# GpSimd starts the work of a head pair after PV of the pair before it, and splits x one pair further back

## The reference

```python
scores = scale * np.matmul(q, k.transpose(0, 1, 3, 2))          # 4 x 8 heads, 576 x 576, head size 64
thresh = np.max(scores, axis=-1, keepdims=True) - tau
scores = np.where(scores >= thresh, scores, -1000000000.0)
attn = np.exp(scores - np.max(scores, axis=-1, keepdims=True))
attn = attn / (np.sum(attn, axis=-1, keepdims=True) + 1e-09)
x = np.matmul(attn, v)                                          # laid out as batch, 576, 512
# token and channel mixing
h = np.maximum(x.transpose(0, 2, 1) @ w_tok1, 0.0) @ w_tok2     # 576 -> 256 -> 576
u = x + h.transpose(0, 2, 1)
y = u + np.maximum(u @ w_ch1, 0.0) @ w_ch2                      # 512 -> 1536 -> 512
# gated convolution
h = np.maximum(y @ w_in, 0.0)                                   # 512 -> 1024
conv_out = ...                                                  # three taps along the sequence
out = h * sigmoid(conv_out) @ w_out
```

## Time and profile before

| what | value |
|---|---|
| median of 3 runs | 849.05 us (848.79 to 851.71) |
| the profiled execution | 850.66 us, of which the span of the trace is 848.9 us |
| PE busy / PEld / DVE / ACT / POOL | 97% / 79% / 50% / 49% / 31% |
| the attention stage | from the start to about 360 us |
| one even and one odd body | 40.1 us, from the first `h1l` at 162.88 us to the first `h1l` at 202.97 us |
| mean granted TensorE clock | 0.997 of full speed |

### The profile page before, as it was taken

The page is one execution under the profiler, slowest core; times in us unless marked ns, Lnnn a source line. Parts: engine busy times, 40 slices in busy tenths (PEclk is TensorE's granted clock), DMA queues, the critical chain, the costliest instruction groups (busy, mean ns, idle before and its releaser), DMA issues.

```text
span 848.9 us, 15131 instructions
## 1 busy us (share of the span) xinstructions
PE 824.3 (97%) x5656; PEld 669.5 (79%) x5656; DVE 422.5 (50%) x829; ACT 412.5 (49%) x914; POOL 265.7 (31%) x202
## 2 busy tenths in 40 slices
PE   8999999999999998899999999999999999999998
PEld 4666776767777766788888888888899989898996
DVE  6897878787877774501211211211214819156380
ACT  4887887877878785211211201211114737355461
POOL 0062415142332323470200100120291726428170
PEclk9999999999999999999999999999999999999999
DMA  9311111111111114000000000000320010100101
GB/s 266 111 48 47 48 48 46 46 46 46 46 46 46 50 16 149 1 1 0 1 1 1 0 1 1 1 0 1 128 71 2 1 51 1 45 17 0 49 0 62
DMA packets 20906, 32.70 MB, mean 39 GB/s; under 512 B 4416, under 2 KB 11136, under 8 KB 20864
## 3 DMA queue, kind: packets, MB, share of 16 engines
q1 hardware_dynamic: 20864, 32.13, 11.7%
HBM read 27.41 MB, written 4.72 MB: 38 GB/s over the span
## 4 chain that ended last, share of the span: by engine, by line
PE 84%; DVE 6%; ACT 6%; issue 3%; POOL 0%; ACTq 0%; DVEq 0%; POOLq 0%
PE score L1203 17%; PE score L1318 12%; PE score L999 5%; PE out_t L1218 4%; PE turn_y L1218 4%; PE mixed L1218 4%; PE turn_x L1218 4%; DVE prob L858 4%; PE out_t L1303 4%; PE out_t L1094 4%; PE mixed L1146 3%; PE mixed L1094 3%; PE turn_y L1303 3%; PE mixed L1303 3%; PE turn_x L1303 3%
## 5 line engine op out<-in xcount | busy, mean ns | idle before, releaser
L921 DVE SCALAR_TENSOR_TENSOR h<-score,h 128x512 fp32r<-128x512 f32 (+1 forms) x60 | 38.3, 638 | 243.5 <-ACT h L693 243.5
L693 ACT ACTIVATE h<-score 128x512 fp32r<-128x512 f32 (+1 forms) x60 | 33.3, 555 | 250.5 <-PE score L1203 250.5
L841 DVE TENSOR_SCALAR_CACHE_REDUCE negs<-score,neg_scale 128x576 f32<-128x576 f32 x144 | 112.7, 816 | 58.7 <-PE score L999 34.0
L858 DVE SCALAR_TENSOR_TENSOR prob<-negs,thresh,exps 128x576 f32<-128x576 f32 x144 | 134.2, 964 | 0.3 <-ACT thresh L594 0.3
L591 ACT ACTIVATE exps<-negs,neg_max 128x576 f32<-128x576 f32 x144 | 104.6, 772 | 1.9 <-DVE negs L841 1.5
L999 PE MATMUL score<-qk 64*128 64x288 f32 x512 | 85.5, 434 | 1.6 <-DVE negs L841 1.0
L1203 PE MATMUL score<-uh,w1h 128*128 128x512 f32 (+1 forms) x240 | 86.9, 368 | 0.0
L1203 PE MATMUL score<-uh,w1l 128*128 128x512 f32 (+1 forms) x240 | 86.8, 368 | 0.0
L1203 PE MATMUL score<-ul,w1h 128*128 128x512 f32 (+1 forms) x240 | 86.8, 368 | 0.0
L559 POOL TENSOR_TENSOR zl<-z,zh 128x512 fp32r<-128x512 f32 x32 | 54.2, 1694 | 98.7 <-ACT zh_t L779 98.7
L999 PEld LDWEIGHTS score<-qk 64*128 64x128 f32 x512 | 46.9, 188 | 28.0 <-issue 13.1
(11 more groups left out here) (184 smaller groups left out, 2010.0 us busy)
## 6 DMA issues: line engine op xcount, KB each, us to landing
qk<-in_qk SPq DMA_DIRECT2D x16, 640.0 KB, 3.9
vm<-in_v SPq DMA_DIRECT2D x16, 320.0 KB, 4.2
result<-ostage SPq DMA_DIRECT2D x16, 256.0 KB, 2.1
w1f<-in_moe_w_ch SPq DMA_DIRECT2D x4, 768.0 KB, 10.8
w2f<-in_moe_w_ch SPq DMA_DIRECT2D x4, 768.0 KB, 7.4
wif<-in_moe_w_in SPq DMA_DIRECT2D x1, 2048.0 KB, 7.8
wof<-in_moe_w_out SPq DMA_DIRECT2D x8, 256.0 KB, 2.6
wt2f<-in_moe_w_tok SPq DMA_DIRECT2D x1, 576.0 KB, 9.4
```

The source lines that it names most:

```text
L841: nc.vector.tensor_scalar(negs[:, i, h, :].rearrange("p (c s) -> p c s", c=2), raw_of[h], neg_scale[:, 0:1], None, ALU.mult, ALU.min, accu ...
L858: nc.vector.scalar_tensor_tensor(out=prob[:, i, h * S:(h + 1) * S], in0=negs[:, i, h, :], scalar=thresh[:, i, h:h + 1], in1=exps[i][:, h, ...
L921: nc.vector.scalar_tensor_tensor(out=h3[:, n % RING, 1, 0:w], in0=hidden_banks[n % 4][:, 0:w], scalar=0.0, in1=h3[:, n % RING, 0, 0:w].bit ...
```

## The change

Only GpSimd's instruction stream is changed. In every body from 1 to 16 it first waits for `pv_done` of pair g-1. `split_x` in body g takes pair g-2, not g-1. `rest_of_token` moves from the odd body to the even one after it. `add_u` of pair g-4 stands in the odd body's start and, for the other pair, at the even body's end. The waits of the other engines are as they were: `normalise_short` and `normalise` of pair g-1 still wait for the split of pair g-2.

```diff
--- before.py
+++ after.py
@@ -458,12 +458,14 @@
             xs_hi = sem("xs_hi")
 
             def split_x(at):
-                pair = at.g - 1
-                mine = slice((at.k - 1) % 2 * P, (at.k - 1) % 2 * P + P)
+                pair = at.g - 2
+                mine = slice(at.k % 2 * P, at.k % 2 * P + P)
                 pool.wait_ge(x_done, pair + 1)
                 pool.wait_ge(short_x, pair + 1)
-                if at.hid:
-                    pool.wait_ge(tok_done, at.g - 1)
+                if at.mix:
+                    pool.wait_ge(tok_done, at.g - 2)
+                if 5 <= at.k and at.k % 2 == 1:
+                    pool.wait_ge(tok_done, at.g - 3)
                 pool.nop(nofuse=True)
                 copy(xh[:, :, mine], x32[:, :, :]).then_inc(xs_hi, 1)
                 pool.wait_ge(xs_hi, pair + 1)
@@ -485,7 +487,7 @@
 
             def rest_of_token(at, i):
 
-                pool.wait_ge(hid_left, at.g - 2 + i)
+                pool.wait_ge(hid_left, at.g - 3 + i)
                 pool.nop(nofuse=True)
                 nc.gpsimd.tensor_tensor(h1l[:, i, :], h1f[:, i, :], h1h[:, i, :].bitcast(F32), ALU.subtract) \
                     .then_inc(tok_lo, 1)
@@ -516,14 +518,14 @@
 
             def body(at):
                 g, k = at.g, at.k
-                if at.mix:
+                if at.pv:
+                    pool.wait_ge(pv_done, g)
+                for i in range(KT if at.mix else 0):
+                    rest_of_token(at, i)
+                if k >= 5 and k % 2 == 1:
                     add_u(g - 4)
-                for i in range(KT if at.hid else 0):
-                    rest_of_token(at, i)
-                if at.pv:
+                if 2 <= k < PAIRS + 2:
                     split_x(at)
-                if at.mix:
-                    add_u(g - 3)
                 if k == 1:
                     split_wt(range(NT))
                 if k == 2:
@@ -531,8 +533,11 @@
                         split_weight(wt2h[:, kt, :], wt2l[:, kt, :], wt2f[:, kt, :], wt_split)
                 if k % 2 == 1 and k < 2 * W1_EARLY:
                     split_w1(g // 2, k == 1)
+                if at.mix:
+                    add_u(g - 4)
 
             bodies(pool, body)
+            add_u(PAIRS - 1)
 
             for c in range(W1_EARLY, KC):
                 split_w1(c, False)
```

## The result

| | median | ratio to before, 95% interval |
|---|---|---|
| before | 849.72 us | |
| after | 872.15 us (872.0 to 872.38, 4 runs) | 1.0261 (1.0241 to 1.0281) |

The profiled execution of the changed kernel has a span of 870.6 us, 21.7 us more than before, at a mean granted clock of 0.988 where it was 0.997. Lines of kernel.py from about 470 on have moved by 2, those from about 540 on by 5: the mask is line 863, PE's turn 1030, PV's last part 1107, `turn_tails` 1084, the short tile 667.

A forecast was written before the change was run, and what follows sets the result against it. PE was taken as the bound, busy 97%. Terms: -2.3 (step 0 masks) + 14.1 (bodies 4 to 15) + 3.9 (body 16) = +15.7 us on a median of 849.05, giving 865 us, range 854 to 874.

The forecast's parts named there:

- Direction and mechanism: Slower (0.84): behind PV, `xl` holds off tile 3's second mask for a whole instruction, and PE waits for that mask.
- Odd body, +1.3 us: Odd bodies, 4 to 15: the second mask ends at 200.1, so `turn_tails` starts at 200.69, not 199.38: +1.3 us each.
- Even body, +1.05 us: Even bodies, 4 to 15: PE gets tile 3's second mask at about 180.75, not 179.70: +1.05 us each.
- What is removed, -2.3 us: Step 0: GpSimd's work leaves the masks there, giving back PE's mask waits from 80 to 320 us: -2.3 us in all.
- Body 16, +3.9 us: Body 16: DVE's split of u and GpSimd's `h1l` take turns, delaying `h1l` and ACT's short tile: +3.9 us.
- Bodies 1 to 3, 0 us: Bodies 1 to 3: split's wait covered, masks may slip, a low clock stretch may not return: 0, between -1.7 and +2.6.
- the rival with 0.04: New stalls bring the lower clock back in every second body, 10 us on top: 875 us and over, chance 0.04.
- The other order at the lock: Tile 3's masks come ahead of `xh` and `xl`, ACT waits 1.75 (even) or 2.05 us (odd): 873 us, chance 0.16.

The follow-up runs named there:

- f4_two_x32_halves: The changed kernel with two buffers x32, one for each parity of the pair, and `xl` made by two instructions: 858.19 us, ratio 1.0101.
- g4_body1_after_x: The changed kernel, with GpSimd in body 1 also waiting for x of pair 0 before it splits the token weights: 867.48 us, ratio 1.0204.
- f3_two_x32: The changed kernel with two buffers x32, one for each parity of the pair, `xl` still one instruction: 869.12 us, ratio 1.0219.
- g3_body16_no_wait: The changed kernel without GpSimd's wait for `pv_done` in body 16 alone: 864.70 us, ratio 1.0191.
- f1_no_pv_wait: The changed kernel without GpSimd's wait for `pv_done` in any body, its new order of instructions kept: 860.43 us, ratio 1.0128.
- g2_before_all_halves: The kernel before with `xl`, the early weight chunks and the second token weight's rests each made in two instructions: 845.90 us, ratio 0.9954.
- h2_change_mended: The changed kernel with two buffers x32, `xl` in two instructions, no `pv_done` wait in body 16, body 1's weights behind x: 850.13 us, ratio 1.0003.

## Why the prediction was right, and where it was off

The forecast was 865 us, the range 854 to 874, the result 872.15. The mechanism was the forecast one; that the number still fell into the range owes something to luck, since the forecast's sum was 2.4 us too high and the clock, which the range left out, added 8.4 us. Point by point:

- **Direction and mechanism: right.** The second mask of tile 3 lasts 2.08 us (2.1 forecast), and PE waits 0.8 and 1.6 us for it, in 11 of the 12 bodies. f4_two_x32_halves shows that the length of `xl` is what the mask waits for, which the Trainium skill's page "SBUF — State Buffer" (section "SBUF: two separate sides") calls a lock for the whole instruction; the numbers agree with it.
- **Odd body, +1.3 us: right.** From the `turn_tails` of body 12 to that of body 13 the delay grows by 1.3 us (260.31 to 272.46, and 279.57 to 293.04). It is right in the sum: the second part of tile 3 starts 1.8 us later, not 1.6, because GpSimd started later than I took, and PE's old wait of 0.24 us for ACT covers as much.
- **Even body, +1.05 us: too high.** It slips by 0.8 us (11.20 to 11.98 for body 12 in the table). PE's second part of tile 3 starts 1.0 us late, and 0.2 us of that had been a wait of PE for ACT's tail drain before, just behind `turn_tails`, which the delay covers. The profile has that wait at a weight load, and I counted waits of the matmuls alone.
- **What is removed, -2.3 us: too small.** The wait for masks in step 1 of the even body was 0.36 us, and 0.52 us a body pair come back. So a pair of bodies costs 1.5 us and not 1.97; six pairs 9 us, not 11.8.
- **Body 16, +3.9 us: the collision is right, the size near.** DVE's two subtractions and the two `h1l` take turns; the last `h1l` ends 3.5 us behind PV (3.84 forecast), `mix_out` starts at 350.81, 2.6 us later than the 15.75 us of this body's PV would make it (2.9 forecast), and ACT's short tile at 353.25, 3.6 us later (3.9 forecast). About 1 us of it comes back in the two bodies behind: the 5.95 us from here to the end, less 3.4 for the clock, are 2.6 us.
- **Bodies 1 to 3, 0 us: off by 1.7.** The step looked at the split alone. What moved was the weights: without a split of pair 0 ahead of them they start 8 us earlier, at 37.6 and not at 45.6 us, and those that follow meet the masks of step 4 (the second lasts 1.81 us and not 0.94). g4_body1_after_x brings PV of body 2 back.
- **The clock: the rival with 0.04 happened, beside the forecast's mechanism.** It had been kept apart from it with a price of 10 us. There are four stretches of 1.7 us and one of 12 x 0.28 = 3.4 us, 10.1 in all, against 1.7 before: 8.4 us. I held it unlikely because PE's waits of 0.4 to 0.5 us left the clock at 1.00; the new waits are three times as long.
- **The sum in rows:** 9 (bodies) + 1.7 (first bodies) + 2.6 (body 16) + 8.4 (clock) = 21.7 us, the difference of the spans. The forecast's 15.7 was 2.4 too high for what it counted (13.3), and left out the clock.
- **The other order at the lock** occurred in one body of twelve, body 5, so that its 873 us is near the result by chance. There `turn_tails` starts at 123.62 us and not at 119.21, 4.41 us later, 2.52 of them from the bodies before: 1.9 us, where that rival had 2.05. I had taken it for all bodies or none. In the other odd bodies it was close. In body 13 GpSimd needed 0.49 us from the end of PV to its start, not the 0.15 us I had read from two instructions of GpSimd's own, and `xh` at 289.15 met a mask issued at 289.14, which still had to wait for it (1.33 us).

## What to carry to other kernels

When work of a side engine is moved, place it against the other engine's instructions that share its way to memory, one by one, also in the variants that take something away: here both the wait and the new order alone put the same 1.5 us instruction in front of a mask that PE needs, in different steps. Splitting a long GpSimd instruction in two costs little (2.52 us with a mask of 0.6 us in between, for 1.85) and bounds what anybody can wait for it; that alone was worth 0.5% in the kernel before. And where PE is the bound, price a new wait of one to two microseconds with the clock that it may cost behind it.

## What the runs showed of the hardware that I had not expected

- Behind waits of PE of 1.6 us the granted clock fell in about half of the cases to the lower of its two levels, for a few microseconds: in the changed kernel behind those of bodies 5, 9 and 15 (windows at 122, 206 and 334 us, 0.79 over 8 us), but not behind equal waits in bodies 7, 11 and 13. In the four profiles with such waits (also f3_two_x32, g3_body16_no_wait, g4_body1_after_x) 12 of 23 have a stretch at or behind them, and all four waits of 2.3 us in body 16 do (the fourth is f4_two_x32_halves). Shorter waits can have one behind them too: f1_no_pv_wait has no stretch behind its waits of 0.9 us in bodies 4 to 16, but the kernel before has one behind a wait of 0.7 us (66 us), and f4_two_x32_halves (321 us), g2_before_all_halves (314 us) and h2_change_mended (318 us) have one behind waits of 0.8 to 0.9 us. That the waits bring the clock down is read from where the stretches lie; what decides between equal waits stays open, and no run here tried it.
- A stretch costs 1.7 us, and whether it comes differs from one execution to the next of the same kernel (h2_change_mended: five at 0.999 to 1.000, five at 0.997 to 0.998).
- GpSimd's start behind an event of PE is not one number. In the changed kernel it is 0.23 us in even bodies of the loop (266.30 + 0.65 to 267.18) and 0.49 us in odd ones, where sequencer instructions stand between the wait and the addition, but 0.75 us in body 5, with the same instructions, and 0.17 us in body 15. What makes body 5 differ stays open; it was enough to turn the order of masks and split.
- The two engines take turns where both have work waiting: in body 16 DVE's two subtractions last 1.23 and 1.75 us and the two `h1l` 1.67 and 1.70 us, each held for the one issued before it.
